# Token product by contraction halves, and two transpositions moved behind the first channel product

## The reference, cut to what matters

```
xt = x.transpose(0, 2, 1)                       # x: the attention's output
h  = np.maximum(xt @ w_tok1, 0.0) @ w_tok2      # 768 -> 256 -> 768, over the tokens
u  = x + h.transpose(0, 2, 1)
h2 = np.maximum(u @ w_ch1, 0.0) @ w_ch2         # 320 -> 1536 -> 320, over the channels
return (u + h2).astype(np.float32)
```

## Time and profile before

| what | us |
|---|---|
| median of 3 runs | 482.42 |
| the 3 runs | 481.11, 482.42, 489.01 |
| the profiled execution | 483.04 |
| its span | 481.3 |
| TensorE busy in it | 453.1 (94%) |
| VectorE, ScalarE, GpSimd busy | 287.2, 228.3, 157.1 |

### The profile page before, as it was taken

One profiled execution on the slowest core, in us unless ns is written; L12 is line 12 of the kernel. 1 busy time (PEld: TensorE's weight loads), 2 busy tenths in 40 slices (PEclk: granted clock), 3 DMA queues, 4 the chain that ended last, 5 costly groups with the idle time before them and its releaser, 6 DMA issues.

```text
span 481.3 us, 9414 instructions
## 1 busy us (share of the span) xinstructions
PE 453.1 (94%) x3408; PEld 417.0 (87%) x3408; DVE 287.2 (60%) x660; ACT 228.3 (47%) x564; POOL 157.1 (33%) x212
## 2 busy tenths in 40 slices
PE   4987998798999999899999999899999999999996
PEld 2765787697999999789999999799999998899996
DVE  7586656788887415677887425577887324411312
ACT  2745347955656224865665224865555212212111
POOL 2435233445664101366655101366654000000000
PEclk9997699889999999999999999899999999999999
DMA  7798588144444301344444301344331001000101
GB/s 215 203 276 247 161 249 290 40 125 134 131 132 140 113 0 43 114 133 134 134 132 142 108 1 44 110 134 135 133 103 43 1 1 42 1 0 1 42 0 41
DMA packets 39189, 50.91 MB, mean 106 GB/s; under 512 B 3554, under 2 KB 31016, under 8 KB 39144
## 3 DMA queue, kind: packets, MB, share of 16 engines
q1 hardware_dynamic: 39144, 50.32, 34.6%
HBM read 46.27 MB, written 4.03 MB: 105 GB/s over the span
## 4 chain that ended last, share of the span: by engine, by line
PE 83%; DVE 5%; ACT 5%; issue 3%; DMA 2%; SPq 1%; DVEq 0%; ACTq 0%
PE pC L951 30%; PE pS L871 6%; PE pA L1023 6%; PE pA L1024 6%; PE pA L1025 6%; PE pA L951 4%; PE pY L928 4%; PE pA L1027 3%; PE pA L1028 3%; PE pY L909 3%; PE pN L885 2%; PE pC L839 2%; DMA wc_raw<-w_ch_dram 2%; PE pC L871 1%; PE pY L918 1%
## 5 line engine op out<-in xcount | busy, mean ns | idle before, releaser
L812 DVE SCALAR_TENSOR_TENSOR h_lo<-pA,h_hi 128x384 fp32r<-128x384 f32 x96 | 53.2, 554 | 117.8 <-ACT h_hi L614 117.8
L614 ACT ACTIVATE h_hi<-pA 128x384 fp32r<-128x384 f32 x96 | 46.7, 487 | 133.5 <-PE pA L1028 133.5
L951 PE MATMUL pC<-wc_hi,h_hi 128*128 128x320 f32 x288 | 94.1, 327 | 0.1
L951 PE MATMUL pC<-wc_lo,h_hi 128*128 128x320 f32 x288 | 89.2, 310 | 0.0
L951 PE MATMUL pC<-wc_hi,h_lo 128*128 128x320 f32 x288 | 88.9, 309 | 0.0
L421 POOL TENSOR_TENSOR gb<-gb,pb 128x384 f32<-128x384 f32 (+1 forms) x54 | 46.3, 857 | 111.5 <-ACT pb L528 111.2
L1023 PE MATMUL pA<-uT_hi,wc_hi 128*128 128x384 f32 x192 | 65.8, 343 | 2.5 <-DVE uT_hi L790 2.5
L518 ACT ACTIVATE gb<-gb,aT 128x128 f32<-128x128 f32 x192 | 62.9, 389 | 7.0 <-POOL gb L432 6.9
L1024 PE MATMUL pA<-uT_lo,wc_hi 128*128 128x384 f32 x192 | 65.2, 340 | 0.0
L1025 PE MATMUL pA<-uT_hi,wc_lo 128*128 128x384 f32 x192 | 64.9, 338 | 0.0
L697 DVE TENSOR_TENSOR pb<-gb,pb 128x384 bf16<-128x384 f32 (+1 forms) x54 | 45.4, 840 | 16.6 <-ACT pb L534 15.5
(11 more groups left out here) (113 smaller groups left out, 876.1 us busy)
## 6 DMA issues: line engine op xcount, KB each, us to landing
gb<-g_dram SPq DMA_DIRECT2D x23, 512.0 KB, 3.9
kv<-kvN_dram SPq DMA_DIRECT2D x24, 324.0 KB, 4.9
kd<-kT_dram SPq DMA_DIRECT2D x24, 180.0 KB
qz<-qT_dram SPq DMA_DIRECT2D x72, 60.0 KB
out_dram<-u SPq DMA_DIRECT2D x24, 160.0 KB, 1.9
gq<-g_dram SPq DMA_DIRECT2D x60, 60.0 KB
qd<-qT_dram SPq DMA_DIRECT2D x20, 180.0 KB, 5.0
x<-o_gate_dram SPq DMA_DIRECT2D x4, 640.0 KB, 4.5
```

Of the source, the lines that this page charges most:

```text
L614: nc.scalar.activation(h2[0][:, slot % 2], pA[slot % 2][:, 0:HALF], ACT.Relu).then_inc(h2_hi, 1)
L812: nc.vector.scalar_tensor_tensor(h2[1][:, slot % 2], pA[slot % 2][:, 0:HALF], 0.0, h2[0][:, slot % 2].bitcast(F32), ALU.max, ALU.subtract) ...
L951: ins = mm(dst, a[p], b[q], start=first and n == 0, stop=last and n == 2)
```

## The change

The second token product of the tiles 0 to 2 runs by halves of the contraction: the first half of all three, then the second half of all three, with the transposition of tile 0 behind them. Tile s from 3 on is followed by the transposition of tile s - 2 (before: s - 1). The last two transpositions (tiles 4 and 5) go to the first channel slot, one ahead of the attention's step and one behind it, and write `pC[0]` and `pC[1]`. ACT and DVE take their splits there too, around their share of that step; the sigmoid moves from ahead of ACT's share to behind the last high split. hidden(0) and hidden(1) wait for the low splits of tiles 2 and 3, project(0) for all.

```
--- before.py
+++ after.py
@@ -147,6 +147,10 @@
         def scores_bank(ba, m):
 
             return [pS, pC[0], pC[1]][m % NG] if ba == 0 else pS
+
+        def transposed_bank(s):
+
+            return pA[s % 2] if s < NC - 2 else pC[s - (NC - 2)]
 
         def values_bank(ba, c):
 
@@ -588,17 +592,17 @@
                     nc.scalar.activation(h1[0][:, m], pA[m][:, 0:DM], ACT.Relu).then_inc(h1_hi, 1)
                 if more:
                     attention(b + 1, 0)
-                for s in range(NC + 1):
-                    if s < NC:
-                        act.wait_ge(u_ready, NC * b + s + 1)
-                        nc.scalar.activation(u[:, s, DM:3 * L], u[:, s, 2 * L:DM], ACT.Copy).then_inc(u_twice, 1)
-                    if s == 0:
-                        continue
-                    s -= 1
+                def u_high(s):
                     act.wait_ge(uT_mm, NC * b + s + 1)
-                    src = pA[s % 2][:, 0:3 * L].rearrange("p (t s) -> p t s", t=3)
+                    src = transposed_bank(s)[:, 0:3 * L].rearrange("p (t s) -> p t s", t=3)
                     nc.scalar.activation(uh[:, :, s * L:(s + 1) * L], src, ACT.Copy).then_inc(uT_hi, 1)
-                    if more and s + 1 == SECOND_AT:
+
+                for s in range(NC):
+                    act.wait_ge(u_ready, NC * b + s + 1)
+                    nc.scalar.activation(u[:, s, DM:3 * L], u[:, s, 2 * L:DM], ACT.Copy).then_inc(u_twice, 1)
+                    if s >= 2:
+                        u_high(s - 2)
+                    if more and s == SECOND_AT:
                         attention(b + 1, 1)
                 if more:
 
@@ -615,10 +619,14 @@
                     if b == 0:
                         for n in slot_pieces(slot):
                             split_hi(n)
-                    if more and slot == 0:
-                        sigmoid(b + 1)
+                    if slot == 0:
+                        u_high(NC - 2)
                     if more:
                         attention(b + 1, slot + AHEAD)
+                    if slot == 0:
+                        u_high(NC - 1)
+                        if more:
+                            sigmoid(b + 1)
 
             for b in range(B):
                 batch(b, b < B - 1)
@@ -785,9 +793,10 @@
                 def u_low(s):
                     dve.wait_ge(uT_hi, NC * b + s + 1)
                     cols = slice(s * L, (s + 1) * L)
-                    nc.vector.tensor_tensor(ul[:, :, cols], pA[s % 2][:, 0:2 * L].rearrange("p (t s) -> p t s", t=2),
+                    bank_s = transposed_bank(s)
+                    nc.vector.tensor_tensor(ul[:, :, cols], bank_s[:, 0:2 * L].rearrange("p (t s) -> p t s", t=2),
                                             uh[:, 0:2, cols].bitcast(F32), ALU.subtract).then_inc(uT_lo, 1)
-                    nc.vector.tensor_tensor(uh[64:128, 2, cols], pA[s % 2][64:128, 2 * L:3 * L],
+                    nc.vector.tensor_tensor(uh[64:128, 2, cols], bank_s[64:128, 2 * L:3 * L],
                                             uh[64:128, 2, cols].bitcast(F32), ALU.subtract).then_inc(uT_lo, 1)
 
                 if more:
@@ -803,8 +812,6 @@
                         attention(b + 1, 1)
                 if more:
                     p_low(b + 1, 0)
-                for s in range(NC - 2, NC):
-                    u_low(s)
                 for slot in range(SLOTS + 1):
                     k = SLOTS * b + slot
                     if slot < SLOTS:
@@ -812,11 +819,15 @@
                         nc.vector.scalar_tensor_tensor(h2[1][:, slot % 2], pA[slot % 2][:, 0:HALF], 0.0,
                                                        h2[0][:, slot % 2].bitcast(F32),
                                                        ALU.max, ALU.subtract).then_inc(h2_lo, 1)
+                    if slot == 0:
+                        u_low(NC - 2)
                     if b == 0:
                         for n in slot_pieces(slot):
                             split_lo(n)
                     if more and slot < SLOTS:
                         attention(b + 1, slot + AHEAD)
+                    if slot == 0:
+                        u_low(NC - 1)
                     if slot == NJ or slot == SLOTS:
                         half = slot // NJ - 1
                         dve.wait_ge(c2_mm, SLOTS * b + slot)
@@ -973,38 +984,44 @@
 
                 def transposes(s):
 
+                    bank_s = transposed_bank(s)
                     pe.wait_ge(u_ready, NC * b + s + 1)
-                    if s >= 2:
+                    if s < 2:
+                        pe.wait_ge(h1_lo, MT * b + s + 1)
+                    elif s < NC - 2:
                         pe.wait_ge(uT_lo, 2 * (NC * b + s - 1))
-                    else:
-                        pe.wait_ge(h1_lo, MT * b + s + 1)
                     for t in range(2):
-                        nc.tensor.transpose(pA[s % 2][:, t * L:(t + 1) * L], u[:, s, t * L:(t + 1) * L], ident[:, :])
+                        nc.tensor.transpose(bank_s[:, t * L:(t + 1) * L], u[:, s, t * L:(t + 1) * L], ident[:, :])
                     pe.wait_ge(u_twice, NC * b + s + 1)
-                    nc.tensor.transpose(pA[s % 2][:, 2 * L:3 * L], u[:, s, 2 * L:3 * L], ident[:, :]).then_inc(uT_mm, 1)
+                    nc.tensor.transpose(bank_s[:, 2 * L:3 * L], u[:, s, 2 * L:3 * L], ident[:, :]).then_inc(uT_mm, 1)
 
                 if more:
                     attention(b + 1, 0)
 
-                for s in range(NC):
-                    if s < ST:
-                        if b != 0:
-                            pe.wait_ge(out_ready, 2 * ST * b)
-                    else:
-                        pe.wait_ge(u_ready, NC * b + s - ST + 1)
+                def mixed(s, m):
+
+                    return split_products(pC[s % ST][:, 0:DM], [w[:, m, s * L:(s + 1) * L] for w in wt2],
+                                          [a[:, m] for a in h1], m == 0, m == MT - 1)
+
+                if b != 0:
+                    pe.wait_ge(out_ready, 2 * ST * b)
+                for m in range(MT):
+                    pe.wait_ge(h1_lo, MT * b + m + 1)
+                    if b == 0:
+                        pe.wait_ge(w_lo, 2 + m + 1)
+                    for s in range(ST):
+                        ins = mixed(s, m)
+                        if m == MT - 1:
+                            ins.then_inc(t2_mm, 1)
+                transposes(0)
+                for s in range(ST, NC):
+                    pe.wait_ge(u_ready, NC * b + s - ST + 1)
                     for m in range(MT):
-                        if s == 0:
-                            pe.wait_ge(h1_lo, MT * b + m + 1)
-                            if b == 0:
-                                pe.wait_ge(w_lo, 2 + m + 1)
-                        ins = split_products(pC[s % ST][:, 0:DM], [w[:, m, s * L:(s + 1) * L] for w in wt2],
-                                             [a[:, m] for a in h1], m == 0, m == MT - 1)
+                        ins = mixed(s, m)
                     ins.then_inc(t2_mm, 1)
-                    if s >= 1:
-                        transposes(s - 1)
+                    transposes(s - 2)
                     if more and s == SECOND_AT:
                         attention(b + 1, 1)
-                transposes(NC - 1)
 
                 def hidden(slot):
 
@@ -1013,7 +1030,9 @@
                     cols = slice(half * HALF, (half + 1) * HALF)
                     f = slice(j * L, (j + 1) * L)
                     if slot < 2:
-                        pe.wait_ge(uT_lo, 2 * (NC * b + NC - 1 + slot))
+                        pe.wait_ge(uT_lo, 2 * (NC * b + ST + slot))
+                    if half == 1 and j == 0:
+                        pe.wait_ge(uT_lo, 2 * NC * (b + 1))
                     if slot >= 2:
                         pe.wait_ge(h2_lo, k - 1)
                     if b == 0 and half == 0 and j % 6 == 0:
@@ -1032,6 +1051,8 @@
                     half, j = divmod(slot, NJ)
                     k = SLOTS * b + slot
                     pe.wait_ge(h2_lo, k + 1)
+                    if j == 0 and half == 0:
+                        pe.wait_ge(uT_lo, 2 * NC * (b + 1))
                     if j == 0 and half == 1:
                         pe.wait_ge(out_ready, 2 * ST * b + ST)
                     if b == 0 and half == 0 and j % 2 == 0:
@@ -1044,8 +1065,12 @@
                 for slot in range(SLOTS + 1):
                     if slot < SLOTS:
                         hidden(slot)
+                    if slot == 0:
+                        transposes(NC - 2)
                     if more and slot < SLOTS:
                         attention(b + 1, slot + AHEAD)
+                    if slot == 0:
+                        transposes(NC - 1)
                     if slot >= 1:
                         project(slot - 1)
 
```

## The result

The changed kernel is slower: 499.96 us median (495.63 to 501.78, four runs) against 485.23 of the kernel before beside it, ratio 1.034, 95% interval 1.027 to 1.041. In a second session: 498.44 against 485.71 (six runs and 29), ratio 1.032 (1.026 to 1.038). Forecast were 491.5, with a range to 497. A kernel's executions differ by up to 3% from one to the next: medians are over all of them, while each ratio compares only those that lie within 1.5% of the fastest of their kernel.

What follows compares the result with a forecast made beforehand. TensorE was busy 94%, but ScalarE was taken to set the pace in the first slots. Terms of +8.8 us on 483.04 gave 491.8, 491.2 after the median's 0.6, taken as 491.5; range 486 to 497.

Steps and rivals of the forecast that it cites:

- The ring: Token stage: addition, copy, high split and low split wait on each other through VectorE and ScalarE, 1.99 us per tile.
- The wait before hidden(0): End of the token stage, second batch: TensorE stands 2 us in one piece after the last token matmul.
- The cover: First slot: ScalarE's queue hides hidden(0)'s earlier start; first Relu 0.34 us later, ScalarE idle 1.4 us for the scores.
- the second Relu: ScalarE, first slots: starts later by 4.0 us in batch 1, 2.46 in batch 2; batch 3 costs 1.9 to 2.5.
- The last batch: No attention or sigmoid: hidden(0) wins 1.2 us, project(0) loses 1.4 waiting for tile 5's low split; about +0.1.
- The queues' sum: Batches 1 to 3 and the last: 4.0 + 2.5 + 2.2 + 0.1 = +8.8 us.
- Both rivals on the other side: Sigmoid's new place in the first slot is covered: 479.7 us, chance 0.12; token stage's waits vanish: 476.4 us, chance 0.06.
- The median of the runs is 0.6 below that execution.: Base of the forecast: the kernel before's profiled execution, 483.04 us, less 0.6, turning 491.8 into 491.2.
- As the clock can only add, I take 491.5.: Last step of the forecast: 491.2 us raised to 491.5 for TensorE's clock.
- a rival at 0.18: Lower clock after TensorE's waits in the three attention batches, up to 1.7 us each: 493 to 497 us, chance 0.18.

Runs made afterwards that it cites:

- Opening the ring alone: Changed kernel with ScalarE's high split s - 2 ahead of copy s in the token stage: 487.59 us, ratio 1.005 to the kernel before.
- The filled wait: Changed kernel with eight unused bf16 matmuls of 512 columns in TensorE's wait before hidden(0): 496.79 us, ratio 1.029 to the kernel before.
- the two orders: Changed kernel with one ScalarE edit each: token stage, high split ahead of copy, 487.59 us; first slot, high splits and sigmoid ahead of attention's share, 488.66 us.
- the lighter sigmoid: Changed kernel with the gate's sigmoid replaced by an exponential, so no table is loaded between; output not the reference's: 486.17 us, ratio 1.011.
- both orders and the tangent: Changed kernel with ScalarE reordered in token stage and first slot, sigmoid written by tanh: 476.73 us, ratio 0.990; another session 477.88, 0.986.
- ScalarE's order of the first slot: Changed kernel with both high splits and the sigmoid ahead of the attention's share in the first slot: 488.66 us, ratio 1.007.

## Why the prediction was wrong

The mechanism of the queues was forecast right, the time was not: it came out at 499.96, 3 us above the range.

- **The ring:** forecast 1.99 us per tile, measured 1.98. The wait before hidden(0): forecast 2, measured 2.05. Hidden(0) was to come 1.1 us earlier in the second batch, and does, once the batch's later start is taken off. Opening the ring alone takes 1.26 us off the wait.
- **The cover:** the first Relu of the slot 0.34 later, measured 0.27; ScalarE standing for 1.4, measured 1.36; the second Relu 4.0, 2.5 and 1.9 to 2.5 later, measured 4.0, 2.5 and 1.87. From hidden(0) to it 9.1, measured 9.14.
- **The last batch,** +0.1: in the three executions where its clock stays at 1.00 it is +0.3 to +0.55.
- **The queues' sum** is therefore 8.65 us, where 8.8 was forecast. Both rivals on the other side fell: nothing of the slot was covered (the Relus 6.03 us apart, not under 5), and the stage's waits did not vanish.

Two steps failed, both in the part that followed the sum.

*"The median of the runs is 0.6 below that execution."* The three runs shown had 482.42. The 69 runs of the kernel before in the sessions of the experiments have a median of 484.84 and reach from 478.60 to 491.61. The profiled execution was not above the median but 1.8 us below it. With the first four runs' median, 485.23, the sum would have been 494.0, still 6 us short: the base is the smaller of the two steps. Counting only the executions within 1.5% of the fastest it is smaller yet: 45 of the 69, with a median of 483.35.

*"As the clock can only add, I take 491.5."* It was put at 0.3 us and as a rival at 0.18. In the profiled execution it took 1.35 us in the third batch and 1.15 in the last, and this execution was the fastest of its four and had the highest mean clock, 0.972; the others had 0.952, 0.959 and 0.952. Over the runs of all kernels, each against its own kernel's mean, 0.01 less of mean clock goes with 2.6 us more (correlation -0.73). The ten runs of the change have a mean of 0.958, the 69 of before 0.972: by that slope, as an estimate, 3.7 us of the 14.2 between their medians. With the queues' 8.65 that leaves some 2 us that no run here explains. The slope comes from the scatter within kernels and need not hold between two of them, so the clock's share is argued and not shown. The rival was right in kind, and it left out the last batch: that has no attention's slots, but it has hidden(0)'s wait, and TensorE is full behind it. What the Trainium skill states in TensorE: Matmul & The Clock Gate, Part 1, that little activity lowers the clock, was weighed as a small chance against the sum. The filled wait is in line with it, in one profile and in the mean clock of six executions; that the same waits are followed by the lower clock in some executions and not in others, no run here accounts for.

The range failed for the same two reasons: it was built round a base 2.4 to 2.8 us under the median of more runs, and ended where the clock's rival did, at 497.

The experiments that take waits away point the same way. Each of the two orders gives back 6.3 us in the profile and 12 to 13 by the ratios, each within about 4; the lighter sigmoid gives 8.8 and 10. So for the two orders a typical execution gains more than the profiles show. The profiled execution of the change was the fastest of its six, 5.2 us under their median, and those above it have a lower mean clock: 0.952 to 0.959, against its 0.962.

## What to carry to other kernels

When two in-order engines hand a tile to each other several times, write out for one tile the chain of who stands behind whom; if it comes back to its start, its length is the time per tile, however idle both engines are, and swapping two instructions in one of the queues can open it. Work moved into a slot should stand ahead of that slot's waits for another engine, not behind one. And where an edit makes TensorE stand for 2 us in one piece, put into the forecast what a lower clock behind it would cost (here 1.15 and 1.35 us where it came), and take the base from as many runs as there are, with their scatter in the range.

## What the runs showed that was not expected

**Two profiles of one kernel differ largely ahead of batch 1.** The kernel with both orders and the tangent was profiled twice, with spans of 478.8 and 473.6 us. Busy time by stretch, the slower execution first:

```profile
40.00:60.00 20.00, 17.05 (x80) 12.58 (x80) 17.16 (x48) 8.74 (x24) 5.26 (x8) 0.74 0.72 203
60.00:80.00 20.00, 18.52 (x94) 16.85 (x95) 6.25 (x16) 7.23 (x22) 5.76 (x8) 0.74 0.74 239
```

```profile
40.00:60.00 20.00, 17.25 (x74) 13.29 (x74) 15.04 (x41) 8.94 (x23) 5.54 (x9) 0.66 0.67 186
60.00:80.00 20.00, 19.19 (x127) 16.80 (x126) 11.66 (x33) 11.01 (x32) 6.97 (x11) 1.00 0.93 293
```

In the slower one a second stretch at the lower clock, 0.74, follows the first, TensorE does 94 instructions in place of 127, and batch 1 begins 4.4 us later (78.78 against 74.35). From there on the two differ by 0.8 us. The profile of the kernel with the ring opened also has a second stretch, 0.57 and then 0.83 in these windows (its batch 1 begins at 78.43) and is the reason why its span, 490.0, looked no better than the change's 491.5.

**The same wait brings the lower clock in one place and not in another.** Behind the 2.05 us before hidden(0) the clock falls in the third batch and stays at 1.00 in the second; behind the 1.80 us before the values of slot 2 likewise. Both profiles of the change agree on this in these two batches. In the kernels of the experiments with the same 2.05 us the places are others: with the exponential the clock is lower behind it in the second batch and not in the third, with ScalarE's order of the first slot in neither. What decides it is open.
